# One unit in eight reordered on TensorE: a single product of layer 2's second one stays beside layer 1's first product, and the second turn becomes one block

## What is computed

```
w = softmax(weight, axis=-1)                         # 8 heads, 7 taps
x = einsum('hk,bskhg->bshg', w, windows_of(x, 7))    # 8192 x 192
h = x @ w_in                                         # layer 1, first product, 192 -> 2048
g = (a0 + a1*h + a2*h^2 + a3*h^3) / (1 + |b0|*|h| + |b1|*h^2 + 1e-6)
x = g @ w_out                                        # layer 1, second product, 2048 -> 192
r = maximum(x @ w_in2, 0)                            # layer 2, first product
out = (s * r * r + b) @ w_out2                       # layer 2, second product
```

## Time and profile before

| | |
|---|---|
| median of 3 runs | 1232.66 us (1232.06 to 1233.21) |
| the profiled execution | 1233.37 us |
| its span, first to last instruction | 1231.6 us |
| granted TensorE clock, mean | 0.998 |
| PE busy | 1214.4 us, 99% |
| DVE and ACT busy | 1080.1 us and 1080.2 us, 88% each |

### The profile page before, as it was taken

The page is one execution under the profiler, slowest core; times in us unless marked ns, Lnnn a source line. Parts: engine busy times, 40 slices in busy tenths (PEclk is TensorE's granted clock), DMA queues, the critical chain, the costliest instruction groups (busy, mean ns, idle before and its releaser), DMA issues.

```text
span 1231.6 us, 25449 instructions
## 1 busy us (share of the span) xinstructions
PE 1214.4 (99%) x10848; PEld 1081.5 (88%) x10848; DVE 1080.1 (88%) x957; ACT 1080.2 (88%) x1128; POOL 383.3 (31%) x196
## 2 busy tenths in 40 slices
PE   8898999999999999999999999999999999999999
PEld 5666899999999999999898989999998988989898
DVE  7998899998999989998999989999899998888810
ACT  6998998989889998899989999898998899888843
POOL 3444333234233242232422333233322333232200
PEclk9999999999999999999999999999999999999999
DMA  8100000000000100001000000001000000000000
GB/s 233 59 1 26 2 1 14 2 15 27 14 1 2 40 1 15 1 3 38 1 15 1 14 28 1 14 2 31 9 15 1 2 14 1 15 1 14 2 14 14
DMA packets 14833, 21.64 MB, mean 18 GB/s; under 512 B 1792, under 2 KB 9984, under 8 KB 14592
## 3 DMA queue, kind: packets, MB, share of 16 engines
q1 hardware_dynamic: 14576, 20.01, 5.6%
q10 hardware_dynamic: 144, 0.01, 0.0%
HBM read 13.72 MB, written 6.29 MB: 16 GB/s over the span
## 4 chain that ended last, share of the span: by engine, by line
PE 91%; DVE 5%; issue 1%; DMA 1%; SPq 1%; ACT 0%; POOL 0%; DVEq 0%; ACTq 0%; POOLq 0%
PE o L664 24%; PE h L644 20%; PE h L638 19%; PE o L650 14%; PE o_tail L656 8%; PE o L506 3%; DMA raw_w_tail_late<-in_moe_w_in_dram 1%; DVE work L1183 1%; DVE work L1151 1%; DVE work L1190 1%; DVE work L1157 1%; DVE work L1154 1%; PE h L498 0%; PE h L499 0%; PE h L489 0%
## 5 line engine op out<-in xcount | busy, mean ns | idle before, releaser
L446 POOL TENSOR_TENSOR gl<-work,gh 128x1024 fp32r<-128x1024 f32 x126 | 304.4, 2416 | 495.3 <-ACT gh L934 494.0
L664 PE MATMUL o<-v,work 64*128 64x192 f32 x3680 | 353.3, 322 | 0.0
L664 PEld LDWEIGHTS o<-v,work 64*128 64x128 f32 x3680 | 330.0, 186 | 12.4
L924 ACT ACTIVATE work<-h,coef 128x1024 f32<-128x1024 f32 x128 | 154.3, 1205 | 91.7 <-PE h L638 89.5
L1151 DVE SCALAR_TENSOR_TENSOR work<-work,coef,h 128x1024 f32<-128x1024 f32 x128 | 163.7, 1279 | 73.8 <-ACT work L925 72.6
L1194 DVE SCALAR_TENSOR_TENSOR work<-work,coef 128x1024 f32<-128x1024 f32 x128 | 164.4, 1285 | 4.5
L1157 DVE SCALAR_TENSOR_TENSOR work<-work,coef,h 128x1024 f32<-128x1024 f32 x128 | 163.9, 1281 | 4.5
L1183 DVE SCALAR_TENSOR_TENSOR work<-work,coef 128x1024 f32<-128x1024 f32 x128 | 164.7, 1287 | 1.9 <-ACT work L929 1.9
L1190 DVE SCALAR_TENSOR_TENSOR work<-work 128x1024 f32<-128x1024 f32 x128 | 156.8, 1225 | 4.4
L650 PE MATMUL o<-gl,v_hi 64*128 64x512 f32 x460 | 159.6, 387 | 0.0
L961 ACT ACTIVATE work<-h 128x1024 f32<-128x1024 f32 x128 | 130.3, 1018 | 32.1 <-PE h L499 32.1
(11 more groups left out here) (142 smaller groups left out, 2713.0 us busy)
## 6 DMA issues: line engine op xcount, KB each, us to landing
out_dram<-y_out SPq DMA_DIRECT2D x32, 192.0 KB, 2.1
xt<-in_x_main_dram SPq DMA_DIRECT2D x7, 518.0 KB, 4.6
xt_tail<-in_x_tail_dram SPq DMA_DIRECT2D x8, 259.0 KB, 4.7
work<-in_moe_w_out_dram SPq DMA_DIRECT2D x2, 768.0 KB, 8.7
v<-in_moe_w_out_dram SPq DMA_DIRECT2D x1, 1536.0 KB, 7.2
raw_w_tail_late<-in_moe_w_in_dram SPq DMA_DIRECT2D x4, 256.0 KB, 7.0
work<-in_moe_w_in_dram SPq DMA_DIRECT2D x2, 512.0 KB, 8.6
xt<-in_x_main_dram SPq DMA_DIRECT2D x2, 259.0 KB, 6.6
```

Of the source, the lines that this page charges most:

```text
L446: nc.gpsimd.tensor_tensor(gl[:, j % 2, :], r_buf[j % 2], gh[:, j % 2, :].bitcast(F32), ALU.subtract).then_inc(gl_ready, 1)
L664: return pe.matmul(o2[:, bank, c, 0:D], g2[buf_out][rows, col:col + P], v2[rows, f, :], start=(f == 0 and c == 0 and upper == (bank == 1)) ...
```

## The change

In `unit_with_sum` four things move, and no instruction is added or taken away:

- Of layer 2's second product only the lower product (bank 0, at 0) stays among layer 1's first product. The lower one at 1 goes behind it. So the lower `first_1(1, False, 0)` now stands right behind the wait for the second `h1_turned`, and `h1_ready` comes from the upper `first_1(0, True, 4)`.
- Three pairs of lower and upper products of the first turn follow as a block.
- The upper `first_2(1, True, 0)` is issued before the second turn instead of behind the wait for `x2_lo`. Both waits for the turns of `o2` now stand ahead of the whole second turn, which is `second_2(1)`.
- Behind the wait for `x2_lo` the upper half has one product less, and `o1_turned` comes from the lower `main_of_second_1(False, 5)` instead of the upper `tail_of_second_1(True, 3)`.

```diff
                     first_1(0, True, 0)
-                    of_second_2(0, False, 1)
-                    first_1(0, True, 1)
                     pe.wait_ge(h1_turned, counted(since * 2 + 2))
+                    for at in range(4):
+                        first_1(1, False, at)
+                        last = first_1(0, True, at + 1)
+                    last.then_inc(h1_ready, 1)
                     for at in range(3):
-                        first_1(1, False, at)
-                        first_1(0, True, at + 2)
-                    first_1(1, False, 3).then_inc(h1_ready, 1)
-                    of_second_2(1, True, 0)
-                    of_second_2(0, False, 2)
-                    of_second_2(1, True, 1)
-                    of_second_2(0, False, 3).then_inc(o2_lower_turned, 1)
-                    of_second_2(1, True, 2)
+                        last = of_second_2(0, False, at + 1)
+                        if at == 2:
+                            last.then_inc(o2_lower_turned, 1)
+                        of_second_2(1, True, at)
...
                     first_2(0, False, 1)
+                    first_2(1, True, 0)
                     pe.wait_ge(o2_lower_turned, counted(t - 1))
-                    of_second_2(0, True, 0)
                     pe.wait_ge(o2_turned, counted(since + 1))
-                    of_second_2(1, False, 0)
-                    for at in range(1, 4):
-                        of_second_2(0, True, at)
-                        last = of_second_2(1, False, at)
-                    last.then_inc(out2_done, 1)
+                    second_2(1).then_inc(out2_done, 1)
...
                     first_2(0, False, 2)
-                    first_2(1, True, 0)
+                    first_2(1, True, 1)
                     main_of_second_1(False, 0)
-                    first_2(1, True, 1)
-                    main_of_second_1(False, 1)
                     first_2(1, True, 2)
-                    for at in range(3):
-                        main_of_second_1(False, at + 2)
+                    for at in range(4):
+                        main_of_second_1(False, at + 1)
                         tail_of_second_1(True, at)
-                    main_of_second_1(False, 5)
-                    tail_of_second_1(True, 3).then_inc(o1_turned, 1)
+                    main_of_second_1(False, 5).then_inc(o1_turned, 1)
```

## The result

| | before | changed |
|---|---|---|
| median, us (22 runs each) | 1232.1 | 1234.0 |
| ratio, with 95% interval | | 1.0013 (1.0008 to 1.0019) |
| the profiled execution's span, us | 1231.6 | 1232.0 |
| unit with a sum, median of 14, us | 9.54 | 9.65 |

The changed kernel is slower by 0.13%, 1.6 us by the ratio (1.0 to 2.3; the medians differ by 1.9). That is inside the 0.2% that I had called no change and inside the wide range, but it is a real loss. It lies outside the 1231.9 to 1233.8 that I gave for the case that x_lo keeps binding, and that case did not happen: x_lo does not bind any more.

A forecast was written before the change was run, and what follows sets the result against it. TensorE's matmul order was taken to bound the kernel, with x_lo binding by 0.11 us in units with a sum. Per unit -0.01 to +0.02, 14 units -0.1 to +0.3, taken as +0.1 on 1232.66: 1232.8 us; range 1231.0 to 1234.8.

The forecast's parts named there:

- the case that x_lo keeps binding: In units with a sum, VectorE's x_lo still holds the load behind it: chance 0.75, range 1231.9 to 1233.8 us.
- the three durations: TensorE products: 512 columns step 0.227 us (0.23 if halves start together), 192 columns take 0.325, passing a wait 0.16.
- the two paths up to x_lo: Upper half nearly back to back, 0.09 us idle at first h1_turned; lower half idle 0.40 us at o2_turned.
- the count of 18 products behind it: Behind x_lo each half has 18 products of 0.2295 us, from 612.40 to the next unit at 616.53.
- The h1_turned part: At the second h1_turned: wait passed at 608.35, lower half pays 0.23 us, upper half 0 to 0.01.
- Second turn: Layer 2's second turn: both halves pass o2_turned at 610.88, start at 610.99, and are free at 612.29 to 612.32.
- h1_ready: Signal from upper first_1(0, True, 4) comes 0.1 us earlier but buys nothing, since ScalarE's L924 starts behind L961.
- B: Slower rival: the held lower load at second h1_turned delays the upper half; 0.24 x 14 = 3.4 us, 1236.1; chance 0.07.
- A: Faster rival: one upper product less behind x_lo shortens units; 0.227 x 14 = 3.2 us, 1229.5; chance 0.08.
- C: First turn's block: program order per record shifts the upper half 0.16; 1.0 us, 1233.8; chance 0.10 with other small costs.
- the four that I had named for being right: Units 9.55 us; load 0.05 after x_lo; lower first_1(1, False, 0) 0.23 after its half frees; L924 starts as L961 ends.
- h1_turned's bubble beyond the margin: Upper bound: bubble of 0.23 not fully absorbed beyond margin 0.09; 0.03 to 0.14 us per unit, up to 2.0 us, 1234.7.

The follow-up runs named there:

- b_short: The kernel before with VectorE adding only the first 256 of 512 columns of the tail sum: 0.9985 times the kernel before, 1230.63 us.
- b_order: The kernel before with VectorE computing x_lo ahead of the rounding of the tail: 0.9996 times the kernel before, 1232.36 against 1232.21 us.
- a_swap: The changed kernel with upper first_1(1, True, 4) issued ahead of lower of_second_2(0, False, 0): 1.0003 times the kernel before, 1232.54 against 1232.36 us.
- o2_only: The kernel before with only the diff's last two hunks (upper first_2 and both o2 waits ahead of the second turn, o1_turned from the lower product): 0.9999, 1232.06 us.
- a_onewait: The changed kernel with the wait for o2_lower_turned moved in front of upper first_2(1, True, 0): 0.9999 times the kernel before, 1232.26 against 1232.36 us.
- a_both: The changed kernel with both the swap of a_swap and the single wait of a_onewait: 0.9999 times the kernel before, 1232.20 against 1232.36 us.

## Why the prediction was right and where it was not

- **The frame held.** The excess of units with a sum, the three durations, the two paths up to x_lo and the count of 18 products behind it are as worked out. x_lo bound the kernel before by 0.11 us (b_short, b_order), and ScalarE's start hung on its own work and not on h1_ready.
- **Step that failed, "The h1_turned part".** It had the wait for the second h1_turned passed at 608.35, 0.05 after its product ended, at a "cost to the upper half 0 to 0.01". It is passed 0.17 after the end, and the upper half pays 0.11 at that place. The trace of before had it too: the held lower product opens at 608.45 in the earlier trace rows, 0.10 after the 608.35 that I had worked out for it, and 0.06 after 608.39, the end of the 192-column product's second record (0.32 after 608.07). I took it for harmless, since its half was still occupied, and did not ask what it waited for. In the kernel before, too, the increment comes 0.12 after its product's end. a_swap showed the cause: the signal comes when the 192-column product issued ahead of the signalling one has ended too, though it runs in the other half. The page "TensorE: Matmul & The Clock Gate" of the Trainium skill, in the part that the prediction drew on, says that matmuls end in program order as well as start in it. I weighed the start and left the end out. By the rule the signal comes at 607.71 in unit 67 of the changed kernel, and 0.07 later the load is seen: for the signal the trace agrees. The matmul records do not show the order, for the signalling product's opens 0.01 before the other's and closes 0.10 before it, by ends that the profile only models.
- **Step that failed, "Second turn".** It let both halves pass o2_turned at 610.88 at no cost for a second wait ahead of it. Two waits in a row put the one for o2_turned into an instruction of its own (51 ns); the load came 0.12 instead of 0.06 after the signal, and the lower half started another 0.03 behind the upper. Together 0.11 us on the last record (o2_only), of which a_onewait gave 0.09 back.
- **Step that failed, "h1_ready".** It was to come 0.1 us earlier. It comes 0.02 later in the unit (increment at 2.70 for 2.68), because the upper half had lost its 0.11 by then. This cost nothing.
- **The sum.** 0.11 + 0.11 is 0.22 us late, less the margin of 0.10 to 0.11: 0.11 to 0.12 per unit, 14 times 1.5 to 1.7 us. The units in the two traces of the changed kernel are 0.11 and 0.09 us longer (1.5 and 1.2 us in all), and the timed loss is 1.6. I had -0.01 to +0.02 per unit.
- **The rivals.** B (slower: the held lower load holds the upper half) named the place and the mechanism of one half of the loss, a wait passed later than worked out with a margin behind it, and put 0.33 late where 0.22 was measured, so it came out beyond 0.2% and the kernel did not. A did not happen: the upper half has a product less behind x_lo, and the unit still ends by the lower half's 18. C is out: the first turn as a block shifts nothing, the upper half's records start with the lower's. In the changed kernel's unit 67 the first records of the block open within 0.01 us of each other in the two halves, so the rule of program order, taken to the start of each record, does not hold there.
- **The signs.** Of the four that I had named for being right, only L924's start (L915 in the changed kernel) held. The units are 9.65 us and not 9.55, the load behind x_lo starts 0.12 after x_lo's end and not 0.05, and the lower first_1(1, False, 0) really starts 0.33 and not 0.23 after its half is free.
- **The range** reached to 1234.8 for h1_turned's bubble beyond the margin (its upper bound of 0.14 us per unit is the whole bubble of 0.23 less 0.09, not the half that the text names). That the measured time fell inside it was luck: the case that I held most likely did not happen. The bubble was indeed the greater unknown, but it was not the idle 0.23 of the lower half, which was absorbed as worked out; it was 0.11 on the upper path, which has no slack.

## What to carry to other kernels

Where several waits feed one critical point, add the delays of the paths before comparing them with the slack: here delays of 0.12 and 0.11 are each about the size of the margin of 0.10 to 0.11 and cost nothing alone, and together they cost 0.11 in each unit. When two halves of the array work side by side, what counts for a signal is all that was issued ahead of it; issue the signalling product first. Where several waits stand in a row, see which of them the trace puts on the held instruction and which into one of its own. And when the trace of the kernel before shows a wait passed later than your rule gives, find out what it waited for before you take its cover away.

## What was new about the hardware

- A signal on a matmul does not come before the end of the product issued before it, also where that one runs in the other half of the array: the increment came 0.12 us after the signalling product's end, and the held load started 0.16 to 0.17 after it, with a product that ended later issued ahead; with the order reversed it was 0.01 and 0.06 (medians of 14 units).
- With two waits in front of one load, the second became a separate wait instruction of 51 ns on TensorE's queue. When that was the wait that came last, the load started 0.12 us after the signal instead of 0.06, although the first wait's product had ended 0.33 us before that of the second; at x_lo's load, where the wait that came last stands on the load, the load starts 0.05 us after x_lo's end with three more waits ahead of it.
- Traces of kernels that are the same up to unit 13 differ by up to 2.0 us there (113.4 to 115.4 us, a_swap and a_both); from unit 13 to 127 one kernel taken twice differed by 0.6 us (1039.68 and 1039.06).
